# Block 0's up product one pair sooner, and penalties one pair in front of their use

## Chip, cores, metric

One core of a Trainium2 chip runs the program. The metric is the device time of one launch in microseconds (us); a median of 3 runs is given. Profiles are of one execution.

## What is computed

The reference has three stages. For B=2, H=8, S=576, D=64:

```python
scores = scale * np.matmul(q, k.transpose(0, 1, 3, 2))
kth = np.partition(scores, -top_k, axis=-1)[..., -top_k:-top_k + 1]   # top_k = 32
scores = np.where(scores >= kth, scores, -1000000000.0)
attn = softmax(scores); x = attn @ v            # to 1152 rows of 512
h = x @ w_in                                    # 512 x 2048
x = (h * np.cos(h)) @ w_out                     # 2048 x 512
expert_idx = np.argmax(x @ w_gate, axis=1)      # 8 experts, capacity 288 rows
h = np.maximum(disp @ w1[e], 0); y = h @ w2[e]  # per expert, 512 x 1024 x 512
out[i] = gate_w[i] * y[expert_idx[i], pos[i]]
```

(softmax is written out in the reference with a maximum, an exp and a division.)

## The kernel before

The rows are cut into 9 blocks of 128. A block of attention is 4 pairs of heads. Block 4 (`MIXED`) has rows of both batches. Each engine has a program of its own, one instruction stream written by hand; semaphores hold them together, and a wait holds everything behind it on its engine.

For a pair `p` of block `i` (a "tile" is one head, 128 x 576):

- PE makes the scores one block ahead (`scores`, L1205) in the bank `p_s`; ACT copies them to `s_sb` (L843).
- DVE finds the 32nd largest by four `max` and three `match_replace` per head (`pair_top`, L374, L377): 14 instructions a pair.
- POOL makes the biases (`bias`, L672); ACT the penalties (`pens`, L850); POOL subtracts them (`masks`, L678); ACT takes the exp (`exp_tile`, L862) into `probs`.
- PE transposes `probs` in three groups (`transpose_probs`, L1222, groups 0 to 11 in a block); ACT copies each to `probsT` (`copy_pT`, L870); PE multiplies with V (`times_v`, L1243) in `p_o`; after two pairs ACT copies `p_o` to `o_sb` (`copy_o`, L876).

Behind attention, and woven into it, each block goes through the up and the output product, one and two blocks late:

- DVE takes reciprocals of the row sums (`reciprocals`), POOL scales (`normalise`, L690), PE transposes x (`transpose_x`, L1253), ACT copies (`copy_xT`, L881).
- `up_half` (L1281) gives h in 4 chunks of 512 columns, two halves each; ACT reads every chunk twice (`copy_h`, L888, L889). POOL takes the fraction of a turn (`fraction`, L702 to L706), ACT the sine (`cosines`, L894), POOL the product (`gated`, L711), ACT casts its high part (`high_g`, L904), DVE subtracts for the low part (`low_g`, L404).
- `down_half` (L1303 to L1305) multiplies chunks of g with w_out in three passes of high and low parts. ACT and POOL split w_out in block 0 (`high_w_out` L910, `low_w_out` L717). Then y is copied, transposed and gated (`copy_y`, `copy_yT`, `copy_logits`).

In PE's block `i` the slots of the four pairs are filled thus by `part`: pair 0 has chunks 2 and 3 of the output product of block `i-2`, pairs 1 and 2 the four up chunks of block `i-1`, pair 3 output chunks 0 and 1 of block `i-1`. Block 0 has no such work, but two idle products a pair (`keep_warm`); block 1 has no part in pair 0. Exp and sine need different tables of ACT, so that a change between them is an `ACT_TABLE_LOAD`; copies, casts and the penalties' Relu take place under either. After the blocks come the routing and the experts, which the change does not touch.

Bodies called with `up=False` are block 0, with `down=False` block 1; the others are the loop's. In ACT the three are `first_body`, `second_body` and `body`.

Of the kernel before, what the change touches and what calls it, by code (L numbers as in the profile page):

```python
# [25 lines left out]
NBLK = NT // P  # L26
# [30 lines left out]
def build(nc, q_in_d, kt_in, v_in, w_in_d, w_out_d, wg_d, w1_d, w2_d, out):  # L57
    y_d = nc.dram_tensor("y_rows", (NBLK - 2, P, DM), F32, kind="Internal").ap()
    slots_d = nc.dram_tensor("slot_rows", (NSLOT, ROW), F32, kind="Internal").ap()
    with ExitStack() as ctx:  # L60
# [210 lines left out]
        def _(sp):  # L271
# [10 lines left out]

            next_queries(0)
            sp.dma_start(w_out, w_out_d).then_inc(w_out_loaded, 16)
# [73 lines left out]
        def _(dve):  # L358
# [48 lines left out]
            def body(i, up=True, down=True, mixed=False, batch=0, more=True):  # L407

                pair_top(i, 0)
                pair_top(i, 1)  # L410
                if up and not down:
                    reciprocals(i - 1)
                if down:
                    low_g(i - 2, 0)
                    low_g(i - 2, 1)
                pair_top(i, 2)
                if down:
                    low_g(i - 2, 2)
                    low_g(i - 2, 3)
                    reciprocals(i - 1)  # L420
                pair_top(i, 3)

            loops(dve, body)


# [231 lines left out]
        def _(pool):  # L657
# [62 lines left out]
            def body(i, up=True, down=True, mixed=False, batch=0, more=True):  # L720
                first, second = not up, up and not down
                if first:
                    for p in range(1, H // 2):
                        bias(i, p)
                        masks(i, p)
                        low_w_out(2 * p - 2)
                        low_w_out(2 * p - 1)
                    bias(i + 1, 0)
                    masks(i + 1, 0)
                    low_w_out(6)  # L730
                    low_w_out(7)
                    return
                if second:
                    normalise(i - 1)
                    bias(i, 1)
                    masks(i, 1)
                    bias(i, 2)
                    masks(i, 2)
                    fraction(i - 1, 0)
                    fraction(i - 1, 1)  # L740
                    bias(i, 3)
                    gated(i - 1, 0)
                    masks(i, 3)
                    gated(i - 1, 1)
                    fraction(i - 1, 2)
                    fraction(i - 1, 3)
                    gated(i - 1, 2)
                    bias(i + 1, 0)
                    gated(i - 1, 3)
                    masks(i + 1, 0)  # L750
                    bias(i + 1, 1)
                    masks(i + 1, 1)
                    bias(i + 1, 2)
                    return
                normalise(i - 1)
                masks(i, 2)
                bias(i, 3)
                fraction(i - 1, 0)
                masks(i, 3)
                fraction(i - 1, 1)  # L760
                if more:
                    bias(i + 1, 0)
# [4 lines left out]
                if more:  # L767
                    masks(i + 1, 0)
                    bias(i + 1, 1)
                gated(i - 1, 2)  # L770
                gated(i - 1, 3)
                if more:
                    masks(i + 1, 1)
                    bias(i + 1, 2)
# [63 lines left out]
        def _(act):  # L838
# [95 lines left out]
            def first_body(i):  # L934

                for p in range(1, H // 2):
                    copy_pT(i, 3 * p - 3)
                    copy_pT(i, 3 * p - 2)
                    scores(i + 1, p - 1)
                    if p == 3:  # L940
                        copy_o(i, 0)
                    copy_pT(i, 3 * p - 1)
                    pens(i, p)
                    exps(i, p)
                    high_w_out(2 * p - 2)
                    high_w_out(2 * p - 1)
# [6 lines left out]
                exps(i + 1, 0)  # L953
                high_w_out(6)
                high_w_out(7)

            def second_body(i):

                copy_pT(i, 0)
                copy_pT(i, 1)  # L960
                scores(i + 1, 0)
                copy_pT(i, 2)
                copy_xT(i - 1)
                pens(i, 1)
                exps(i, 1)

                copy_pT(i, 3)
                copy_pT(i, 4)
                scores(i + 1, 1)
                pens(i, 2)  # L970
                copy_pT(i, 5)
                copy_h(i - 1, 0)
                exp_tile(i, 4)
                copy_o(i, 0)
                copy_h(i - 1, 1)
                exp_tile(i, 5)

                copy_pT(i, 6)
                copy_pT(i, 7)
# [6 lines left out]
                high_g(i - 1, 0)  # L986
                high_g(i - 1, 1)
                exp_tile(i, 7)

                copy_h(i - 1, 3)  # L990
                copy_pT(i, 9)
                copy_pT(i, 10)
                cosines(i - 1, 1)
                scores(i + 1, 3)
                copy_pT(i, 11)
                pens(i + 1, 0)
                high_g(i - 1, 2)
                copy_o(i, 1)
                high_g(i - 1, 3)
                exps(i + 1, 0)  # L1000
                pens(i + 1, 1)

            def body(i, up=True, down=True, mixed=False, batch=0, more=True):

                first, second = not up, up and not down
                if first:
                    first_body(i)
                    return
                if second:
                    second_body(i)  # L1010
                    return
                copy_pT(i, 0)
                copy_pT(i, 1)
                exp_tile(i, 2)
                if more:
                    scores(i + 1, 0)
                copy_pT(i, 2)
                copy_xT(i - 1)
                exp_tile(i, 3)
                pens(i, 2)  # L1020
                if down:
                    copy_y(i - 2)
                copy_pT(i, 3)
                copy_pT(i, 4)
                exp_tile(i, 4)
# [6 lines left out]
                pens(i, 3)  # L1032
                if down:
                    copy_yT(i - 2)
                copy_o(i, 0)

                copy_h(i - 1, 1)
                copy_pT(i, 6)
                copy_pT(i, 7)
                exp_tile(i, 6)  # L1040
                cosines(i - 1, 0)
                copy_pT(i, 8)
                if more:
                    scores(i + 1, 2)
                copy_h(i - 1, 2)
                high_g(i - 1, 0)
                high_g(i - 1, 1)
                exp_tile(i, 7)

                copy_h(i - 1, 3)  # L1050
                copy_pT(i, 9)
                if more:
                    pens(i + 1, 0)
                cosines(i - 1, 1)
                copy_pT(i, 10)
                if more:
                    scores(i + 1, 3)
                copy_pT(i, 11)
                if more:
                    exp_tile(i + 1, 0)  # L1060
                high_g(i - 1, 2)
                if down:
                    copy_logits(i - 2)
                high_g(i - 1, 3)
                if more:
                    exp_tile(i + 1, 1)
                copy_o(i, 1)
                if more:
                    pens(i + 1, 1)
# [118 lines left out]
        def _(pe):  # L1188
# [145 lines left out]
            def body(i, keys, next_keys, up=True, down=True, mixed=False, batch=0, more=True):  # L1334
                def part(t, half):

                    if t < 2 and down:
                        down_half(i - 2, 2 + t, half)
                    if 2 <= t < 6 and up:
                        up_half(i - 1, t - 2, half)  # L1340
                    if t >= 6 and up:
                        down_half(i - 1, t - 6, half)

                for p in range(H // 2):
# [14 lines left out]
                    if p == 0 and up:  # L1359
# [199 lines left out]
```

## Time and profile before

| what | value |
|---|---|
| median of 3 runs | 661.59 us (660.81 to 661.72) |
| the profiled execution | 662.5 us, span 660.8 us |
| PE busy | 611.5 us, 93% |
| DVE busy | 526.6 us, 80% |
| ACT busy | 437.7 us, 66% |
| POOL busy | 289.7 us, 44% |

The table gives the sum of each engine's instructions over the span. It is a mean over the attention blocks (to about 440 us), the routing and the experts. The chain of waits is by 66% of the span on PE and by 15% on ACT.

### The profile page before, as it was taken

How to read it: one execution, taken by the hardware profiler on the slowest of the kernel's cores; microseconds unless marked ns; L12 is line 12 of the kernel's file. 1: busy time of each engine (PE TensorE's matmuls, PEld its weight loads, DVE VectorE, ACT ScalarE, POOL GpSimd, SP SyncE). 2: the span in 40 equal slices, each digit the busy share in tenths (PEclk: the TensorE clock that was granted, in tenths of full speed). 3: DMA queues.
4: the chain of work that ended last, by engine and by line, in shares of the span. 5: the costliest groups of instructions: out<-in, count | busy, mean ns of one | idle time of the engine just before them, and what ended most of it. 6: DMA issues, size and time to landing. Idle time of an engine off the chain costs nothing.

```text
span 660.8 us, 13481 instructions
## 1 busy us (share of the span) xinstructions
PE 611.5 (93%) x4302; PEld 548.3 (83%) x4302; DVE 526.6 (80%) x1017; ACT 437.7 (66%) x727; POOL 289.7 (44%) x294
## 2 busy tenths in 40 slices
PE   4778798899999999999999999999898999999994
PEld 3556696798897898998988978989687999999994
DVE  5999999988989979989989985016539877789751
ACT  2567478679679679688596796736438665667630
POOL 0376559457477366566474675821500111011111
PEclk9988599999999999999999999999899999999998
DMA  5874700000000000000000000060398675675400
GB/s 180 354 325 172 270 5 5 26 5 5 25 5 5 25 6 5 25 9 1 28 4 16 0 0 18 1 235 5 144 348 303 231 269 199 248 248 221 147 18 16
DMA packets 17792, 68.62 MB, mean 104 GB/s; under 512 B 1998, under 2 KB 6606, under 8 KB 15056
## 3 DMA queue, kind: packets, MB, share of 16 engines
q1 hardware_dynamic: 16000, 63.27, 25.8%
q0 software_dynamic: 1744, 4.73, 2.0%
q8 instruction: 27, 0.44, 0.3%
q14 instruction: 21, 0.17, 0.1%
HBM read 54.33 MB, written 14.45 MB: 104 GB/s over the span
## 4 chain that ended last, share of the span: by engine, by line
PE 66%; ACT 15%; POOL 8%; issue 7%; DVE 3%; DMA 0%; POOLq 0%; ACTq 0%; SPq 0%; DVEq 0%
PE p_a L1281 8%; PE p_o L1243 6%; PE p_b L1281 5%; PE p_s L1205 5%; PE p_b L1303 4%; PE p_t L1222 3%; PE p_s L1498 3%; PE p_b L1305 3%; PE p_b L1304 3%; PE p_t L1498 3%; PE p_t L1475 3%; POOL arena L678 3%; PE p_s L1475 3%; ACT arena L843 2%; POOL w_out_lo L717 2%
## 5 line engine op out<-in xcount | busy, mean ns | idle before, releaser
L374 DVE MAX8 top<-arena 128x8 f32<-128x576 f32 x288 | 201.1, 745 | 7.4 <-ACT arena L843 7.3
L377 DVE MATCH_REPLACE8 arena<-top,arena 128x576 f32<-128x576 f32 x216 | 158.6, 741 | 0.0
L678 POOL TENSOR_TENSOR arena<-arena,pen 128x576 f32<-128x576 f32 x72 | 100.7, 1421 | 57.1 <-ACT pen L850 57.1
L1243 PEld LDWEIGHTS p_o<-arena,probsT 128*128 128x128 f32 (+1 forms) x720 | 85.7, 191 | 12.8 <-ACT probsT L870 6.8
L1243 PE MATMUL p_o<-arena,probsT 128*128 128x65 f32 (+1 forms) x720 | 90.9, 273 | 5.6 <-ACT probsT L870 3.8
L870 ACT COPY probsT<-p_t 128x384 f32<-128x384 f32 x108 | 51.3, 480 | 53.9 <-PE p_t L1222 53.8
L1222 PE MATMUL p_t<-ident,arena 128*128 128x128 f32 x324 | 55.7, 284 | 13.2 <-ACT arena L862 13.2
L1281 PE MATMUL p_a<-xT,wff 128*128 128x128 f32 x512 | 66.0, 283 | 0.0
L1281 PE MATMUL p_b<-xT,wff 128*128 128x128 f32 x512 | 64.3, 279 | 0.0
L1303 PE MATMUL p_b<-w_out_lo,g_hi 128*128 128x512 f32 x144 | 62.5, 434 | 1.9 <-ACT h_sb L889 1.6
L1281 PEld LDWEIGHTS p_a<-xT,wff 128*128 128x128 f32 x512 | 60.8, 195 | 2.8 <-issue 2.4
L1222 PEld LDWEIGHTS p_t<-ident,arena 128*128 128x128 f32 x324 | 41.6, 148 | 24.7 <-ACT arena L862 17.8
L862 ACT ACTIVATE arena<-arena,biases 128x576 f32<-128x576 f32 x72 | 56.0, 779 | 9.1 <-POOL arena L678 8.3
L404 DVE TENSOR_TENSOR g_lo<-h_sb,g_hi 128x512 fp32r<-128x512 f32 x36 | 27.9, 811 | 42.0 <-ACT g_hi L904 41.6
L1281 PEld LDWEIGHTS p_b<-xT,wff 128*128 128x128 f32 x512 | 59.7, 192 | 0.3
L1205 PE MATMUL p_s<-arena,q_sb 64*128 64x160 f32 (+3 forms) x320 | 51.6, 476 | 8.4 <-DMA arena<-in_kt 4.3
L1305 PE MATMUL p_b<-w_out_hi,g_lo 128*128 128x512 f32 x144 | 56.7, 394 | 0.0
L1304 PE MATMUL p_b<-w_out_hi,g_hi 128*128 128x512 f32 x144 | 56.5, 392 | 0.0
L1205 PEld LDWEIGHTS p_s<-arena,q_sb 64*128 64x128 f32 (+1 forms) x320 | 36.8, 195 | 20.0 <-issue 17.0
L850 ACT ACTIVATE pen<-arena,biases 128x576 f32<-128x576 f32 x72 | 52.0, 776 | 1.6 <-POOL biases L672 1.6
L843 ACT COPY arena<-p_s 128x576 f32<-128x576 f32 x72 | 42.4, 644 | 14.2 <-PE p_s L1205 14.2
L711 POOL TENSOR_TENSOR h_sb<-h_sb,turns 128x512 f32<-128x512 f32 x32 | 40.5, 1285 | 23.0 <-ACT turns L894 23.0
(186 smaller groups left out, 1309.4 us busy)
## 6 DMA issues: line engine op xcount, KB each, us to landing
arena<-in_w SPq DMA_DIRECT2D x8, 2048.0 KB, 9.0
wff<-in_w SPq DMA_DIRECT2D x8, 2048.0 KB, 9.1
slot_rows<-y_now SPq DMA_DIRECT2D x1, 4626.0 KB, 14.7
wff<-in_w_out SPq DMA_DIRECT2D x1, 4096.0 KB, 12.2
wff<-in_w_in SPq DMA_DIRECT2D x1, 4096.0 KB, 22.0
wff<-slot_rows SPq DMA_DIRECT2D x8, 385.5 KB, 3.7
arena<-in_vones SPq DMA_DIRECT2D x2, 1300.0 KB, 16.8
q_sb<-in_q SPq DMA_DIRECT2D x36, 64.0 KB, 1.9
```

What stands on the lines that cost most here:

```text
L374: nc.vector.max(best, src).then_inc(top_step, 1)
L377: nc.vector.match_replace(work[:, a, :], best, src, LOWEST).then_inc(top_step, 1)
L678: nc.gpsimd.tensor_tensor(s_sb[:, t, :], s_sb[:, t, :], pen[:, t % 2, :], ALU.subtract).then_inc(masked, 1)
L843: nc.scalar.copy(s_sb[:, t, :], p_s[:, SPOT[t % 2]:SPOT[t % 2] + S]).then_inc(scores_copied, 1)
L862: nc.scalar.activation(probs[:, S * (t % 2):S * (t % 2) + S], s_sb[:, t, :], ACT.Exp, bias=biases[:, t, 0:1], scale=SCALE).then_inc(probs_ ...
L1205: last = mm(p_s[q, at + lo:at + hi], q_sb[d, p, q], kT[d, b, p, lo:hi], start=True, stop=True)
L1222: last = nc.tensor.transpose(p_t[:, at:at + P], probs[:, k:k + P], ident[:])
L1243: last = mm(p_o[q, lo:lo + n], probsT[:, g % 2, P * c + q.start:P * c + q.stop], vones[b][:, p, at:at + n], start=(k == 0), stop=(k == PAI ...
L1281: last = mm(bank_c[:, P * n:P * n + P], w_in[:, k, P * f:P * f + P], xT[:, k, :], start=(k == 0), stop=(k == KC - 1))
L1303: mm(p_b[:], g_hi[:, cols], w_out_lo[:, f, :], start=(f == 0), stop=False)
L1304: mm(p_b[:], g_hi[:, cols], w_out_hi[:, f, :], start=False, stop=False)
L1305: last = mm(p_b[:], g_lo[:, cols], w_out_hi[:, f, :], start=False, stop=(f == FC1 - 1))
```

## The change

Nothing is added or taken out: every engine has the same instructions in another order.

1. PE, block 1: the transpose of block 0's x stands first in the block, and up chunks 0 to 3 fill pairs 0 and 1; pair 2 has attention alone. Other blocks are as before.
2. ACT, POOL and DVE, all loop blocks: penalties, masks and top-k of a pair come one pair later against PE (`pens(i, 1)` to `pens(i, 3)` in pairs 0 to 2, `pens(i + 1, 0)` in pair 3), low parts and reciprocals one pair of top-k sooner. The sines stand before exp tile 6 and before the next block's exp tile 0.
3. Block 0: w_out is loaded before the queries of block 1, and its casts and low parts are shared out anew.

The core of the diff:

```diff
@@ sync
+            sp.dma_start(w_out, w_out_d).then_inc(w_out_loaded, 16)
             next_queries(0)
-            sp.dma_start(w_out, w_out_d).then_inc(w_out_loaded, 16)
@@ vector, loop body
                 pair_top(i, 0)
+                low_g(i - 2, 0)
+                low_g(i - 2, 1)
                 pair_top(i, 1)
...
+                low_g(i - 2, 2)
+                low_g(i - 2, 3)
+                reciprocals(i - 1)
                 pair_top(i, 2)
...
                 pair_top(i, 3)
@@ vector, block 1
+            pair_top(1, 0)
+            pair_top(1, 1, range(0, 2))
+            reciprocals(0)
+            pair_top(1, 1, range(2, 7))
@@ gpsimd, block 0
+                    low_w_out(0)
+                    low_w_out(1)
+                    bias(i, 1)
+                    masks(i, 1)
+                    low_w_out(2)
+                    low_w_out(3)
+                    bias(i, 2)
+                    masks(i, 2)
+                    bias(i, 3)
+                    masks(i, 3)
+                    low_w_out(4)
+                    low_w_out(5)
                     bias(i + 1, 0)
@@ gpsimd, block 1
                     normalise(i - 1)
+                    masks(i, 0)
+                    low_w_out(6)
+                    low_w_out(7)
@@ scalar, block 1
+                copy_xT(i - 1)
+                exps(i, 0)
...
                 copy_o(i, 0)
-                copy_h(i - 1, 1)
-                exp_tile(i, 5)
+                cosines(i - 1, 0)
+                exps(i, 2)
+                copy_h(i - 1, 2)
+                high_g(i - 1, 0)
+                high_g(i - 1, 1)
                 copy_pT(i, 6)
+                copy_h(i - 1, 3)
+                scores(i + 1, 2)
                 copy_pT(i, 7)
-                scores(i + 1, 2)
-                cosines(i - 1, 0)
                 pens(i, 3)
                 copy_pT(i, 8)
-                copy_h(i - 1, 2)
-                exp_tile(i, 6)
...
+                exps(i, 3)
@@ scalar, loop body
                 copy_pT(i, 7)
-                exp_tile(i, 6)
-                cosines(i - 1, 0)
-                copy_pT(i, 8)
                 if more:
                     scores(i + 1, 2)
+                pens(i, 3)
+                copy_pT(i, 8)
                 copy_h(i - 1, 2)
+                cosines(i - 1, 0)
+                exp_tile(i, 6)
                 high_g(i - 1, 0)
+                exp_tile(i, 7)
                 high_g(i - 1, 1)
...
@@ tensor
-                    if 2 <= t < 6 and up:
-                        up_half(i - 1, t - 2, half)
+                    c = t - 2 if down else t
+                    if 0 <= c < 4 and up:
+                        up_half(i - 1, c, half)
...
+                if up and not down:
+                    transpose_x(i - 1)
```

In the changed file the lines of the engines stand 7 to 11 further down.

ACT, pair 2 of block 4 (the same in all loop blocks), before: `p_t` copies are the transposes 6, 7 and 8, `arena<-arena,biases` is an exp tile, `turns<-turns` a sine.

```order
L870 COPY probsT<-p_t 128x384 x2
L862 ACTIVATE arena<-arena,biases 128x576
L894 ACT_TABLE_LOAD
L894 ACTIVATE turns<-turns 128x512 x2
L870 COPY probsT<-p_t 128x384
L843 COPY arena<-p_s 128x576 x2
L888 ACTIVATE turns<-p_a 128x512
L889 COPY h_sb<-p_a 128x512
L904 CAST g_hi<-h_sb 128x512 x2
L862 ACT_TABLE_LOAD
L862 ACTIVATE arena<-arena,biases 128x576
```

ACT, the same place in the changed kernel:

```order
L877 COPY probsT<-p_t 128x384 x2
L850 COPY arena<-p_s 128x576 x2
L857 ACTIVATE pen<-arena,biases 128x576 x2
L877 COPY probsT<-p_t 128x384
L895 ACTIVATE turns<-p_a 128x512
L896 COPY h_sb<-p_a 128x512
L901 ACT_TABLE_LOAD
L901 ACTIVATE turns<-turns 128x512 x2
L869 ACT_TABLE_LOAD
L869 ACTIVATE arena<-arena,biases 128x576
L911 CAST g_hi<-h_sb 128x512
L869 ACTIVATE arena<-arena,biases 128x576
```

The exp tile between transposes 7 and the sines (tile 6) stands behind the sines and a second table load now.

ACT, the end of block 4, before:

```order
L870 COPY probsT<-p_t 128x384
L850 ACTIVATE pen<-arena,biases 128x576 x2
L894 ACT_TABLE_LOAD
L894 ACTIVATE turns<-turns 128x512 x2
L870 COPY probsT<-p_t 128x384
L843 COPY arena<-p_s 128x576 x2
L870 COPY probsT<-p_t 128x384
L862 ACT_TABLE_LOAD
L862 ACTIVATE arena<-arena,biases 128x576
L904 CAST g_hi<-h_sb 128x512
```

ACT, the end of block 4 in the changed kernel:

```order
L877 COPY probsT<-p_t 128x384 x2
L850 COPY arena<-p_s 128x576 x2
L857 ACTIVATE pen<-arena,biases 128x576 x2
L937 COPY logits<-p_a 128x8
L877 COPY probsT<-p_t 128x384
L901 ACT_TABLE_LOAD
L901 ACTIVATE turns<-turns 128x512 x2
L869 ACT_TABLE_LOAD
L869 ACTIVATE arena<-arena,biases 128x576
L911 CAST g_hi<-h_sb 128x512
L883 COPY o_sb<-p_o 128x260
```

The copies of transposes 10 and 11 and the scores stood between the sines and the next block's exp tile 0; they are all in front of the sines now, and exp tile 0 comes straight behind them.

PE, start of block 1 before (`p_a<-ident,odd_whole` transposes x, `p_b<-arena` are the idle products of block 0):

```order
L1373 MATMUL p_b<-arena 128x512 x2
L1222 MATMUL p_t<-ident,arena 128x128 x3
L1205 MATMUL p_s<-arena,q_sb 128x160
L1205 MATMUL p_s<-arena,q_sb 128x416 x2
L1205 MATMUL p_s<-arena,q_sb 128x160
L1222 MATMUL p_t<-ident,arena 128x128 x3
L1243 MATMUL p_o<-arena,probsT 128x65 x3
L1222 MATMUL p_t<-ident,arena 128x128 x3
L1253 MATMUL p_a<-ident,odd_whole 128x128 x4
```

PE, start of block 1 in the changed kernel:

```order
L1384 MATMUL p_b<-arena 128x512 x2
L1260 MATMUL p_a<-ident,odd_whole 128x128 x4
L1229 MATMUL p_t<-ident,arena 128x128 x3
L1212 MATMUL p_s<-arena,q_sb 128x160
L1212 MATMUL p_s<-arena,q_sb 128x416 x2
L1212 MATMUL p_s<-arena,q_sb 128x160
L1288 MATMUL p_a<-xT,wff 128x128 x8
L1229 MATMUL p_t<-ident,arena 128x128 x3
L1250 MATMUL p_o<-arena,probsT 128x65 x3
L1288 MATMUL p_a<-xT,wff 128x128 x8
```

The transpose of x came behind three groups of transposes of `probs` and is the first thing of the block now, with the up product (`p_a<-xT,wff`) right behind the scores.

## Rows read from the trace of the kernel before

**Rows 1.** Busy time of one engine, page part 1: us, share, instructions.
```profile
PE 611.5 (93%) x4302; PEld 548.3 (83%) x4302; DVE 526.6 (80%) x1017; ACT 437.7 (66%) x727; POOL 289.7 (44%) x294
```

**Rows 2.** Busy time by stretch: length, then each engine, clock, DMA; blocks 5 and 8.
```profile
256.41:301.88 45.47, 45.07 (x334) 40.64 (x332) 41.44 (x86) 35.26 (x62) 28.28 (x29) 1.00 0.04 13
...
393.69:436.63 42.94, 41.07 (x305) 37.21 (x304) 14.43 (x31) 29.37 (x52) 26.45 (x32) 1.00 0.04 11
```

**Rows 3.** PE timeline, block 5, pairs 2 and 3: start us, us, instruction.
```profile
278.72 0.49 PE L1222 MATMUL p_t<-ident,arena 128*128 128x128 f32 x3
...
283.14 2.00 PE L1281 MATMUL p_a<-xT,wff 128*128 128x128 f32 x16
284.98 0.49 PE L1222 MATMUL p_t<-ident,arena 128*128 128x128 f32 x3
...
290.22 0.49 PE L1222 MATMUL p_t<-ident,arena 128*128 128x128 f32 x3
...
294.40 0.49 PE L1222 MATMUL p_t<-ident,arena 128*128 128x128 f32 x3
...
297.65 0.88 PE L1243 MATMUL p_o<-arena,probsT 128*128 128x65 f32 x6 [0.37 <-ACT probsT L870]
...
301.88 0.49 PE L1222 MATMUL p_t<-ident,arena 128*128 128x128 f32 x3
```

**Rows 4.** ACT timeline, the same stretch.
```profile
282.73 0.48 ACT L870 COPY probsT<-p_t 128x384 f32<-128x384 f32 x1 [2.35 <-PE p_t L1222]
...
283.90 1.28 ACT L894 ACT_TABLE_LOAD   x1
285.19 1.15 ACT L894 ACTIVATE turns<-turns 128x512 f32<-128x512 f32 x2
...
286.61 1.18 ACT L843 COPY arena<-p_s 128x576 f32<-128x576 f32 x2
287.67 0.62 ACT L888 ACTIVATE turns<-p_a 128x512 f32<-128x512 f32 x1
...
288.62 1.18 ACT L904 CAST g_hi<-h_sb 128x512 fp32r<-128x512 f32 x2
...
291.11 0.77 ACT L862 ACTIVATE arena<-arena,biases 128x576 f32<-128x576 f32 x1
...
293.11 1.46 ACT L850 ACTIVATE pen<-arena,biases 128x576 f32<-128x576 f32 x2
```

**Rows 5.** PE timeline before block 2.
```profile
79.69 3.25 PE L1281 MATMUL p_a<-xT,wff 128*128 128x128 f32 x16
...
103.64 0.55 PE L1222 MATMUL p_t<-ident,arena 128*128 128x128 f32 x3 [0.34 <-ACT arena L862]
...
117.50 0.55 PE L1222 MATMUL p_t<-ident,arena 128*128 128x128 f32 x3 [2.41 <-ACT arena L862]
```

**Rows 6.** DVE timeline, end of a pair of top-k and first low halves.
```profile
102.72 1.41 DVE L374 MAX8 top<-arena 128x8 f32<-128x576 f32 x2
104.24 1.71 DVE L404 TENSOR_TENSOR g_lo<-h_sb,g_hi 128x512 fp32r<-128x512 f32 x2
```

**Rows 7.** POOL timeline, end of block 0.
```profile
66.14 4.68 POOL L717 TENSOR_TENSOR w_out_lo<-wff,w_out_hi 128x1024 fp32r<-128x1024 f32 x2 [1.82 <-ACT w_out_hi L910]
70.78 1.05 POOL L690 TENSOR_TENSOR odd_whole<-o_sb,rden 128x512 f32<-128x512 f32 x1
```

**Rows 8.** ACT timeline, block 0.
```profile
23.06 0.46 ACT L870 COPY probsT<-p_t 128x384 f32<-128x384 f32 x1
...
59.95 0.38 ACT L876 COPY o_sb<-p_o 128x260 f32<-128x260 f32 x1 [0.97 <-PE p_o L1243]
```

**Rows 9.** Busy time by stretch of 4 us, columns as in rows 2.
```profile
40.00:44.00 4.00, 1.54 (x8) 0.62 (x6) 4.00 (x11) 2.55 (x4) 2.78 (x2) 1.00 1.00 419
44.00:48.00 4.00, 2.22 (x12) 1.44 (x11) 4.00 (x8) 3.64 (x7) 3.35 (x2) 0.59 0.49 183
```

**Rows 10.** DMA issues, page part 6: KB each, us to landing.
```profile
wff<-in_w_out SPq DMA_DIRECT2D x1, 4096.0 KB, 12.2
```

More of the change, by code:

```diff
@@ L405, in low_g, with body @@
                                         ALU.subtract).then_inc(g_lo_made, 1)
-            def body(i, up=True, down=True, mixed=False, batch=0, more=True):
+            def body(i):
                 pair_top(i, 0)
+                low_g(i - 2, 0)
+                low_g(i - 2, 1)
                 pair_top(i, 1)
[L411 to L415, printed above, removed]
+                low_g(i - 2, 2)
+                low_g(i - 2, 3)
+                reciprocals(i - 1)
                 pair_top(i, 2)
[L417 to L420, printed above, removed]
                 pair_top(i, 3)
-            loops(dve, body)
+            for p in range(H // 2):
+                pair_top(0, p)
+            pair_top(1, 0)
+            pair_top(1, 1, range(0, 2))
+            reciprocals(0)
+            pair_top(1, 1, range(2, 7))
+            pair_top(1, 2)
+            pair_top(1, 3)
+            with dve.Fori(2, NBLK) as i:
+                body(i)
             steps = [0]
@@ L767, in body @@
                 if more:
+                    bias(i + 1, 0)
                     masks(i + 1, 0)
-                    bias(i + 1, 1)
                 gated(i - 1, 2)
                 gated(i - 1, 3)
-                if more:
-                    masks(i + 1, 1)
-                    bias(i + 1, 2)
             pool.wait_ge(signs_ready, 2)
@@ L934, in first_body @@
             def first_body(i):
[L936 to L946, printed above, removed]
+                high_w_out(0)
+                high_w_out(1)
+                copy_pT(i, 0)
+                copy_pT(i, 1)
+                scores(i + 1, 0)
+                copy_pT(i, 2)
+                pens(i, 1)
+                exps(i, 1)
+                high_w_out(2)
+                high_w_out(3)
+                copy_pT(i, 3)
+                copy_pT(i, 4)
+                scores(i + 1, 1)
+                copy_pT(i, 5)
+                pens(i, 2)
+                exps(i, 2)
+                copy_o(i, 0)
+                copy_pT(i, 6)
+                copy_pT(i, 7)
+                scores(i + 1, 2)
+                copy_pT(i, 8)
+                pens(i, 3)
+                exps(i, 3)
+                high_w_out(4)
+                high_w_out(5)
                 copy_pT(i, 9)
@@ L952, in first_body @@
                 pens(i + 1, 0)
-                exps(i + 1, 0)
                 high_w_out(6)
@@ L1013, in body @@
                 copy_pT(i, 1)
-                exp_tile(i, 2)
                 if more:
                     scores(i + 1, 0)
+                pens(i, 1)
                 copy_pT(i, 2)
                 copy_xT(i - 1)
+                exp_tile(i, 2)
+                copy_y(i - 2)
                 exp_tile(i, 3)
-                pens(i, 2)
-                if down:
-                    copy_y(i - 2)
                 copy_pT(i, 3)
                 copy_pT(i, 4)
-                exp_tile(i, 4)
                 if more:
@@ L1061, in body @@
                 high_g(i - 1, 2)
-                if down:
-                    copy_logits(i - 2)
-                high_g(i - 1, 3)
+                copy_o(i, 1)
                 if more:
                     exp_tile(i + 1, 1)
-                copy_o(i, 1)
-                if more:
-                    pens(i + 1, 1)
+                high_g(i - 1, 3)
             for p in range(H // 2):
@@ L1358, in body @@
                     transpose_probs(i, g + 2)
-                    if p == 0 and up:
+                    if p == 0 and up and down:
                         transpose_x(i - 1)
```

76 lines of the change are left out of this document (32 added, 44 removed).

## The prediction

> **What bounds the kernel now.** I read the busy table of the page first, then the busy time by stretch, one stretch per block, then the timelines of PE and ACT in one block of the loop, and at last the timelines of the first 120 us. PE is busy 611.5 of 660.8 us [rows 1]. In a block of the loop it is busy 45.07 of 45.47 us at granted clock 1.00, while DVE, ACT and POOL have 41.44, 35.26 and 28.28 [rows 2]. So from block 2 to block 8 PE is the bound, and what counts is whether a wait is put in its way. The PE timeline of block 5 shows one: 0.37 us before a product with V at 297.65, released by ACT's copy of the probabilities [rows 3]. Pair 2 of that block lasts 11.50 us (278.72 to 290.22), pair 3 lasts 11.66 us (290.22 to 301.88), 11.3 without its wait. ACT is not the bound by its sum, but it runs in order, and each exp tile stands in front of a group of PE's transposes. In the old order exp tile 6, due at the start of pair 3, is computed before the table load for the sines, and exp tile 0 of the next block comes after sines that start five steps earlier in the pair. Before block 2 it is different: DVE is full, PE is often idle and half of the time at half clock [rows 9].
>
> **The steady blocks, step by step.** The work is the same in kind and count, four table loads per block among it. What moves is ACT's order. In pair 2 it is now: copy of transposes 8, reading of up chunk 2, table load, two sines, table load, exp tile 6. The transposes 8 end at 284.98 + 0.49, which is 6.75 us after the start of the pair [rows 3]. Just then ACT is free in the new order as well: ACT copies transposes 7 from 282.73 on, 4.0 us into the pair, and that copy (0.4), two score tiles (1.06) and two penalties (1.4) bring it to 6.8 [rows 4]. From there: copy 0.4, the two readings of an up chunk 1.05, load 1.28, sines 1.15, load 1.28, exp 0.78, all from [rows 4], sum 5.9. Exp tile 6 is ready at 12.7 us, PE asks for it at 11.5. **A wait of 1.25 us**, in each of blocks 2 to 7. In block 8 PE has no scores to make, so its pair is 1.2 us shorter and the wait about 2.2.
>
> At the end of pair 3 the order is now: copy of transposes 10, scores 3, the penalties of the next block, logits, copy of transposes 11, load, two sines, load, exp tile 0 of the next block. Transposes 10 end at 294.40 + 0.49, 4.7 us into the pair [rows 3]. Then 0.4 + 1.06 + 1.46 + 0.5 + 1.28 + 1.15 + 1.28 + 0.78 = 7.9 [rows 4]: ready at 12.6, asked for at 11.3. **A wait of 1.3 us** at the start of blocks 3 to 8, six times. The present wait of 0.37 us goes, since that copy stands before the sines now. Per block this is 1.25 + 1.3 - 0.37 = 2.2 us, and for blocks 2 to 7 it is +13.1 us. The blocks around the change of batch (3 and 4) have longer products with V, of which some 0.5 us fall into these waits: -0.5. Block 8: +2.2, and about +0.8 because the last sines now stand before the copy of the last output half, on which the last x depends, less 0.2 of the 1.9 us that PE idles there now [rows 2]: +2.8.
>
> The bounds of these terms. Below: if ACT's steps overlapped so that both chains came in time, 0 us per block and the 0.37 gone. Above: POOL's fraction steps and masks share the pairs, and if they came 0.5 us late at each of the two places, another +6 in sum. I take the sums of rows, since every link is a row of its own.
>
> DVE's order by itself is free: it has 41.44 of 45.47 us, now of 47.7, and the low halves, which now stand before top-k of pair 1 instead of pair 2, wait for the casts of g, not for DVE. POOL's sum is free too, but bias 3 comes behind two masks and two fractions now, and is ready about when ACT arrives for the penalties of pair 3. That is a tie without slack; hence the upper bound.
>
> **The first blocks.** The casts of w_out move up. SP issues its 4096 KB before its first wait; they land in 12.2 us [rows 10], and ACT wants them at 23.06 us [rows 8], with nine small loads in front. Price 0; if it were late, ACT would stand with the copies of block 0 behind it, 2 us at most. The queries of block 1 queue behind it, wanted 1 us later. Price 0, bound the same 2 us. Low halves 0 and 1 now stand before POOL's second bias; two of them take 4.7 us [rows 7], from 24.1 to 28.8, and hold that bias 0.3 us past the copy it is anyway behind: 0. DVE's reciprocals of block 0 move into the middle of pair 1; waiting for the copy of o_sb there costs DVE at most 0.5 us, which nobody asks for. Low halves 6 and 7 of w_out take POOL from 66.14 to 70.8 us now, and the x of block 0 waits for that [rows 7]. In the new order x comes first. Its input, the copy of o_sb at 59.95 [rows 8], comes some 1.5 us sooner, since no w_out step stands before the last bias. So x is ready near 60.4 instead of 71.8, two casts, the copy of xT and exp tile 0 follow on ACT, and PE starts block 1 at 63.7. The first up product is at about 66 instead of 79.69 [rows 5].
>
> But PE cannot keep these 14 us. Pairs 0 and 1 with two chunks each take 11.5 us each as in the loop, plus 1.5 to 3.5 us at half clock: the granted clock fell to 0.59 in the stretch after one with PE busy for 1.54 of 4 us [rows 9]. Pair 2 begins near 89 to 90. It has attention alone, 4.1 us of PE (11.5 less four up halves of 1.84, from 283.14 to 284.98 [rows 3]), but ACT has there load, two sines, load, two exps, two chunk readings, two casts, scores, penalties, copies and the exp of tile 6: 1.28 + 1.15 + 1.28 + 1.4 + 1.9 + 1.2 + 1.06 + 1.4 + 1.1 + 0.8 = 12.6 us [rows 4]. Pair 3 begins near 102, 1.6 us before the 103.64 of now [rows 5]. It takes 11.3 us, or up to 14.6 if the clock falls after the thin pair 2. Block 2 starts between 113.3 and 116.6 instead of 117.50. I take **-2 us**. The bounds: DVE reaches the low half of g a pair of top-k earlier (14 instructions at 0.7 us) than its 104.24 [rows 6], so the lead can't exceed some 9.5 us; and if the clock stays down longer, +1.
>
> **Sum.** 13.1 - 0.5 + 2.8 - 2 = +13.4 us. The profiled execution had 662.5 us; that makes 675.9. The median of the runs is 0.9 lower, so 675.0.
>
> A rule against the change stands in the Trainium skill (ScalarE: Activation LUTs, What ACT_TABLE_LOAD costs): a switch costs 1.28 us of load and about 1.38 of drain. By that rule, each of the two chains, with two loads, would be 2.8 us longer, and the kernel an estimated 33 us slower again, above 700. The rows show 1.28 us and then the first sine 1.29 after the load's start [rows 4], so I go by the rows; chance 0.01.
>
> **The rivals.**
> - *The lead is kept* (0.17). Block 2 starts 6 to 9.5 us early, limited by DVE. For it: DVE has no gap, and the new order asks for its results a pair later. Against: ACT's 12.6 us in a pair with 4.1 us of PE. Time: 675 - 4 to 7.5, that is 667.5 to 671.
> - *Faster* (0.08). Both exp tiles come in time, since PE's transposes 8 or the bias come sooner than I read, and the lead is kept as well. It decides at 4.7 us from transposes 8 to the end of exp tile 6, where I add up 5.9. Time: -9.5 - 6 x 0.37 = 650. With half a lead 655.
> - *More waits* (0.12). POOL is late with bias 3, or the casts of g come late for the output chunks, 0.5 to 1 us per block twice: 681 to 687.
> - *It cancels* (0.03): half of the waits and the full lead, near 661.
> - My forecast, both waits and a small lead: 0.59, 671 to 681.
>
> **Numbers.** The range goes from 666, which takes in the full lead with both waits, to 682. About 0.2% can be told from no change. Faster 0.08, same 0.03, slower 0.89.
>
> **What would show it.** In the profile after: block stretches of 47 to 48 us in place of 45.5 to 46.2; PE idle about 1.3 us before the transposes at the start of pair 3 and of pair 0, released by ACT's exp; no wait before the product with V behind transposes 10; the first up product near 66 us; block 2 starting at 113 to 117 us; the expert part as long as before. Wrong it would be if blocks keep 45.5 us, or block 2 starts before 110.

## The result, and the profile after

The changed kernel takes 689.01 us (median of 4 runs, 688.16 to 692.13) beside 661.65 us for the kernel before, measured beside it: a ratio of 1.0412, 95% interval 1.0385 to 1.0439. The profiled execution had 688.6 us, span 686.9 us. The sign was forecast, the size (675.0, at most 682) was not.

The page of the changed kernel, busy time and the chain of waits by engine; the first line answers to [rows 1]:

```profile
PE 620.8 (90%) x4302; PEld 555.0 (81%) x4302; DVE 526.7 (77%) x1017; ACT 440.4 (64%) x727; POOL 291.5 (42%) x294
...
PE 53%; ACT 14%; issue 13%; POOL 12%; DVE 5%; POOLq 1%; DVEq 1%; DMA 0%; ACTq 0%; SPq 0%
```

PE is busy 9.3 us longer with the same 4302 instructions, so some of them ran at a lower clock; the other 17 us of the longer span are time in which PE is idle. Its busy time by stretch, one stretch from the first transposes of a block to those of the next, for blocks 2, 3, 4, 5, 7 and 8 and for the rest (columns as in [rows 2]; the last stretch begins at the last transpose of x):

```profile
115.39:164.27 48.88, 45.20 (x333) 40.48 (x333) 40.15 (x83) 35.21 (x60) 28.51 (x29) 1.00 0.04 12
164.27:214.62 50.35, 46.62 (x364) 40.77 (x364) 41.73 (x86) 36.40 (x63) 28.69 (x31) 0.97 0.04 11
214.62:264.10 49.48, 47.87 (x404) 40.26 (x405) 42.75 (x86) 36.42 (x63) 28.46 (x30) 1.00 0.04 12
264.10:313.06 48.96, 45.20 (x333) 40.48 (x333) 42.07 (x87) 36.40 (x63) 29.15 (x30) 1.00 0.04 12
...
362.02:412.41 50.39, 46.72 (x332) 41.48 (x333) 41.73 (x86) 36.33 (x63) 28.56 (x30) 0.97 0.01 5
412.41:463.27 50.86, 44.25 (x301) 40.33 (x301) 23.97 (x50) 30.20 (x53) 26.75 (x34) 0.90 0.05 17
463.27:686.90 223.63, 209.06 (x1422) 198.36 (x1422) 151.27 (x248) 120.09 (x188) 29.27 (x25) 0.98 0.52 192
```

The same stretches of blocks 3, 4 and 8 in the kernel before, where [rows 2] has block 8 cut 0.6 us later:

```profile
163.02:208.84 45.82, 45.12 (x365) 39.93 (x364) 42.38 (x87) 36.01 (x63) 28.32 (x29) 1.00 0.04 13
208.84:256.41 47.57, 47.57 (x406) 40.23 (x405) 42.51 (x88) 36.92 (x64) 28.56 (x29) 1.00 0.04 13
...
393.69:436.03 42.34, 40.47 (x302) 36.79 (x300) 13.83 (x30) 29.37 (x52) 26.45 (x32) 1.00 0.03 9
```

Block 2 starts at 115.39 us, forecast 113.3 to 116.6 [rows 5]. From there a block takes 48.9 to 49.0 us, block 4 (rows of both batches) 49.5 us, blocks 3 and 7 50.4 us. Before, a block took 45.5 to 45.9 us and block 4 47.6 us. Of blocks 2 to 7 the granted clock is 0.97 in just blocks 3 and 7, and 1.00 in the others. Block 8 takes 50.9 us to the last transpose of x, 8.5 us more than before. What follows is no longer than before (223.6 us, before 224.8).

PE's timeline of block 5, pairs 2 and 3, the same place as [rows 3] (in brackets how long the engine was idle before an instruction, and which engine, tile and line released it):

```profile
286.46 0.49 PE L1229 MATMUL p_t<-ident,arena 128*128 128x128 f32 x3
...
292.73 0.49 PE L1229 MATMUL p_t<-ident,arena 128*128 128x128 f32 x3
...
299.58 0.55 PE L1229 MATMUL p_t<-ident,arena 128*128 128x128 f32 x3 [1.45 <-ACT arena L869]
...
303.74 0.49 PE L1229 MATMUL p_t<-ident,arena 128*128 128x128 f32 x3
...
308.51 0.80 PE L1250 MATMUL p_o<-arena,probsT 128*128 128x65 f32 x6
...
313.06 0.54 PE L1229 MATMUL p_t<-ident,arena 128*128 128x128 f32 x3 [2.30 <-ACT arena L869]
```

The pair-3 transposes come 13.12 us after those of pair 2 and waited 1.45 us for exp tile 6; the first transposes of the next block waited 2.30 us for exp tile 0. The wait before the product with V (297.65 in [rows 3]) is gone. These are the two waits that were forecast, at 1.25 and 1.3 us. ACT's timeline, the same stretch, which answers to [rows 4]:

```profile
292.20 1.44 ACT L857 ACTIVATE pen<-arena,biases 128x576 f32<-128x576 f32 x2 [0.17 <-POOL biases L677]
...
295.00 1.28 ACT L901 ACT_TABLE_LOAD   x1
296.29 1.15 ACT L901 ACTIVATE turns<-turns 128x512 f32<-128x512 f32 x2
297.46 1.28 ACT L869 ACT_TABLE_LOAD   x1
298.75 0.78 ACT L869 ACTIVATE arena<-arena,biases 128x576 f32<-128x576 f32 x1
...
304.26 0.48 ACT L877 COPY probsT<-p_t 128x384 f32<-128x384 f32 x1 [1.70 <-PE p_t L1229]
304.64 1.19 ACT L850 COPY arena<-p_s 128x576 f32<-128x576 f32 x2
306.50 1.44 ACT L857 ACTIVATE pen<-arena,biases 128x576 f32<-128x576 f32 x2 [0.68 <-POOL biases L677]
...
308.39 1.28 ACT L901 ACT_TABLE_LOAD   x1
309.69 1.15 ACT L901 ACTIVATE turns<-turns 128x512 f32<-128x512 f32 x2
310.86 1.28 ACT L869 ACT_TABLE_LOAD   x1
312.15 0.78 ACT L869 ACTIVATE arena<-arena,biases 128x576 f32<-128x576 f32 x1
```

Both chains are there link by link: load 1.28, sines 1.15, load 1.28, exp tile, in pair 2 behind the readings of h, in pair 3 behind the penalties and two short copies. But at 306.50 ACT had waited 0.68 us for POOL's bias. POOL's timeline of pair 3:

```profile
299.56 0.62 POOL L707 TENSOR_SCALAR odd_whole<-turns 128x512 f32<-128x512 f32 x1
...
305.01 1.30 POOL L711 TENSOR_TENSOR turns<-turns,odd_whole 128x512 f32<-128x512 f32 x1 [0.18 <-POOL odd_whole L709]
306.27 0.20 POOL L677 TENSOR_TENSOR biases<-top,signs 128x4 f32<-128x4 f32 x1
307.46 2.82 POOL L683 TENSOR_TENSOR arena<-arena,pen 128x576 f32<-128x576 f32 x2 [0.98 <-ACT pen L857]
```

The bias (306.27) comes behind two fractions (299.56 to 306.3), which themselves start behind the products of the pair before.

The waits of PE in block 8, and before the last transpose of x:

```profile
413.76 0.50 PE L1310 MATMUL p_b<-w_out_lo,g_hi 128*128 128x512 f32 x1 [0.80 <-DVE g_lo L404]
...
447.26 0.55 PE L1229 MATMUL p_t<-ident,arena 128*128 128x128 f32 x3 [2.22 <-ACT arena L869]
...
449.92 0.79 PE L1310 MATMUL p_b<-w_out_lo,g_hi 128*128 128x512 f32 x1 [1.32 <-ACT h_sb L896]
...
463.27 0.66 PE L1260 MATMUL p_a<-ident,odd_whole 128*128 128x128 f32 x4 [2.27 <-DVE odd_whole L512]
```

Four waits of 0.80, 2.22, 1.32 and 2.27 us, 6.6 us together where block 8 had 1.9 us before, and a granted clock of 0.90 over the block.

### The profile page after: what moved, and what is told of

The parts are those of the page before. It is cut to its first block, busy times and chain, and to the rows that moved or that the text cites. A ratio compares the mean times of both kernels' runs of the same rounds, so it can differ in the third digit from the quotient of the medians.

```text
span 686.9 us, 13728 instructions
## 1 busy us (share of the span) xinstructions
PE 620.8 (90%) x4302; PEld 555.0 (81%) x4302; DVE 526.7 (77%) x1017; ACT 440.4 (64%) x727; POOL 291.5 (42%) x294
## 4 chain that ended last, share of the span: by engine, by line
PE 53%; ACT 14%; issue 13%; POOL 12%; DVE 5%; POOLq 1%; DVEq 1%; DMA 0%; ACTq 0%; SPq 0%
PE p_a L1288 5%; PE p_s L1212 5%; PE p_o L1250 4%; PE p_b L1310 3%; PE p_s L1509 3%; PE p_t L1229 3%; PE p_t L1509 3%; PE p_b L1312 3%; PE p_b L1311 3%; PE p_t L1486 3%; POOL arena L683 3%; PE p_s L1486 3%; ACT pen L857 2%; ACT L901 2%; POOL turns L711 2%
## 5 line engine op out<-in xcount | busy, mean ns | idle before, releaser
L1229 PE MATMUL p_t<-ident,arena 128*128 128x128 f32 x324 | 58.2, 293 | 36.4 <-ACT arena L869 36.3
L1310 PE MATMUL p_b<-w_out_lo,g_hi 128*128 128x512 f32 x144 | 65.2, 453 | 2.1 <-ACT h_sb L896 1.3
L1212 PE MATMUL p_s<-arena,q_sb 64*128 64x160 f32 (+3 forms) x320 | 53.5, 492 | 8.4 <-DMA arena<-in_kt 4.3
L1312 PE MATMUL p_b<-w_out_hi,g_lo 128*128 128x512 f32 x144 | 58.8, 409 | 0.0
L1311 PE MATMUL p_b<-w_out_hi,g_hi 128*128 128x512 f32 x144 | 58.7, 408 | 0.0
L828 POOL DMA_INDIRECT out_rows<-turns,own_number x8 | 9.2, 1150 | 94.2 <-DVE turns L601 93.0
```

The costliest lines, as they stand in the source:

```text
L1212: last = mm(p_s[q, at + lo:at + hi], q_sb[d, p, q], kT[d, b, p, lo:hi], start=True, stop=True)
L1229: last = nc.tensor.transpose(p_t[:, at:at + P], probs[:, k:k + P], ident[:])
L1310: mm(p_b[:], g_hi[:, cols], w_out_lo[:, f, :], start=(f == 0), stop=False)
L1311: mm(p_b[:], g_hi[:, cols], w_out_hi[:, f, :], start=False, stop=False)
L1312: last = mm(p_b[:], g_lo[:, cols], w_out_hi[:, f, :], start=False, stop=(f == FC1 - 1))
```

## The experiments

**The start by itself** (`new_start`). Blocks 0 and 1 of the change, the old loop behind them. Beside what the diff of the change has for these blocks, the second bodies end as the old ones did, and DVE makes block 2 in an order between the two:

```diff
@@ vector
+            pair_top(2, 0)
+            low_g(0, 0)
+            low_g(0, 1)
+            pair_top(2, 1)
+            pair_top(2, 2)
+            low_g(0, 2)
+            low_g(0, 3)
+            reciprocals(1)
+            pair_top(2, 3)
@@ gpsimd, end of block 1
+                    bias(i + 1, 1)
+                    masks(i + 1, 1)
+                    bias(i + 1, 2)
@@ scalar, end of block 1
+                pens(i + 1, 1)
```

> Blocks 0 and 1 of the change (all engines, the w_out load first), the old loop from block 2 on, with DVE's low halves of block 0 in their new places. My theory: the blocks of the loop cost the 27 us, and the start by itself gives what the trace of the change shows at the first transposes of block 2, 115.4 instead of 117.5 us: 659.5, 2 us faster than before. Rival, the start also carries a loss that shows later (penalties and top-k of block 2 come late in the old loop): 662 to 665.

Measured: 662.04 us, ratio 0.9999 (0.9982 to 1.0016). Block 2 began even earlier than forecast and PE waited for the low half at once:

```profile
109.80 0.55 PE L1256 MATMUL p_t<-ident,arena 128*128 128x128 f32 x3 [1.18 <-ACT arena L887]
...
115.64 0.77 PE L1337 MATMUL p_b<-w_out_lo,g_hi 128*128 128x512 f32 x1 [4.12 <-DVE g_lo L404]
```

The lead of 7.7 us was there, and 4.1 us of it went in one wait. Behind that wait PE was busy all the time, but at half clock:

```profile
115.64:120.00 4.36, 4.36 (x15) 3.67 (x15) 4.33 (x11) 0.79 (x2) 1.58 (x2) 0.50 0.00 0
```

At 157.61 us, before a product with V in pair 3, PE was 1.2 us ahead of the same place before (158.79). So the start neither costs nor gives anything by itself; the gain that I expected (2 us) is not there, and neither is the rival's loss (the kernel before took 662.33 us beside it).

**The loop by itself** (`new_loop`): the old blocks 0 and 1 in front of the new loop, and nothing at their end for pair 1 and 2 of block 2.

```diff
@@ gpsimd, end of block 1
-                    bias(i + 1, 1)
-                    masks(i + 1, 1)
-                    bias(i + 1, 2)
@@ scalar, end of block 1
-                pens(i + 1, 1)
```

> The old blocks 0 and 1 with the new order of the loop from block 2 on. My theory: all of the loss is here, so 2 us more than the change: 690 to 692. Rival, a part of the loss comes from how block 1 hands over to block 2: 680 or less.

Measured: 693.95 us in one run, 2 us above what I expected. The same waits stand in its trace at the same places (1.48 and 2.31 us in block 5). All of the loss is in the loop's order. From block 2 to the last transpose of x this profile is 3.0 us longer than the one of the change. Its waits there are no longer, but the clock was 0.97 in four of blocks 2 to 7 instead of two.

**An exp tile in front of the sines** (`exp6_first`, `exp0_first`).

```diff
@@ exp6_first, scalar, pair 2
+                exp_tile(i, 6)
                 cosines(i - 1, 0)
-                exp_tile(i, 6)
@@ exp0_first, scalar, pair 3
+                if more:
+                    exp_tile(i + 1, 0)
                 cosines(i - 1, 1)
-                if more:
-                    exp_tile(i + 1, 0)
```

> The change with exp tile 6 in front of the first two sines, nothing else. By the prediction's step (PE waits at pair 3 for that tile alone) the 1.45 us before the transposes of pair 3 go, 7 times: 679. Rival: the sines and the reading of the last up chunk come late as well, and the wait moves to the output product that stands behind them in pair 3: same time within 3 us, and PE waits there 1.5 to 2 us a block, released by the copy of h or the low half of g.

> The change with exp tile 0 of the next block in front of the last two sines, nothing else. By the prediction's step the 2.3 us at the start of a block go, 6 times: 675. Rival: the wait moves to output chunk 2 in pair 0, behind the low half of g: same time within 3 us.

Measured: 695.61 and 694.77 us, one run each, 6.6 and 5.8 us above the median of the change. In each, PE no longer waits for the tile that was moved; it waits at the next output product instead, in block 5 of `exp6_first` here, with what is left of the wait at the start of the next block:

```profile
305.58 0.80 PE L1310 MATMUL p_b<-w_out_lo,g_hi 128*128 128x512 f32 x1 [2.70 <-ACT h_sb L896]
...
317.64 0.54 PE L1229 MATMUL p_t<-ident,arena 128*128 128x128 f32 x3 [1.09 <-ACT arena L869]
```

and at the start of block 6 of `exp0_first` here:

```profile
315.73 0.50 PE L1310 MATMUL p_b<-w_out_lo,g_hi 128*128 128x512 f32 x1 [2.75 <-DVE g_lo L404]
```

2.7 us each, longer than the wait that went (1.45 and 2.30 us). The sum of a block's waits grew less: 3.8 us in `exp6_first` and 4.5 in `exp0_first`, beside 3.75 in the change. The rivals had the mechanism right: what is late is the whole chain with the sines, and whichever tile is put in front of it, the other work behind it (the reading of the last up chunk, the low half of g) becomes what PE waits for. The time was outside their "within 3 us". In `exp6_first` most of the excess is clock: it was 0.93 to 0.97 in every block from 2 to 8, and PE was busy 5.4 us longer there than in the change. In `exp0_first` it is 3.7 us of waits in these blocks, and a later part (routing and experts) that took 3.6 us longer, which the edit doesn't touch.

**The table loads taken away** (`no_sine`, and `before_no_sine` as the control). The sine is replaced by a copy, so that the blocks need one table.

```diff
-                nc.scalar.activation(part, part, ACT.Sin, scale=TURN)
+                nc.scalar.activation(part, part, ACT.Copy, scale=TURN)
```

> The change with ACT's Copy in place of the sine, so that the blocks have no table load. It leaves out the cosine: g is h times the angle, and so the routing of rows to experts can differ; only the blocks (to the last transpose of x) are to be read. My theory: ACT's chain between two exp tiles is 2.6 us shorter at both places, both waits go, and a loop block takes 45 to 45.5 us in place of 48.9 to 50.4. Rival: the new order holds PE also without the loads (POOL's biases and fractions): 47 us or more.

> The kernel before with the same replacement, cosine left out, as the control for no_sine: its blocks keep 45 to 46 us, since PE waits for ACT less than half a microsecond a block there.

Measured: 658.16 and 651.46 us. Read from the transpose of x in block 2 to that in block 8, six blocks: 113.97 to 392.73 is 46.5 us a block with the new order, 120.06 to 390.11 is 45.0 with the old. With the sines the same places give 49.7 (121.25 to 419.57) and 46.1. So of 3.6 us that the new order costs per block, 2.2 hang on the table loads (and on what they do to the clock, which was 1.00 in both kernels without sines) and 1.4 to 1.5 do not. I had expected 45 to 45.5; the rival had a part. What is left is mostly one wait a block, in pair 0 before output chunk 2 (one run each):

```profile
295.91 0.50 PE L1310 MATMUL p_b<-w_out_lo,g_hi 128*128 128x512 f32 x1 [1.08 <-DVE g_lo L404]
```

and POOL's timeline ahead of it shows where the lateness comes from:

```profile
288.84 0.20 POOL L677 TENSOR_TENSOR biases<-top,signs 128x4 f32<-128x4 f32 x1
290.03 2.81 POOL L683 TENSOR_TENSOR arena<-arena,pen 128x576 f32<-128x576 f32 x2 [0.99 <-ACT pen L857]
292.80 2.51 POOL L716 TENSOR_TENSOR h_sb<-h_sb,turns 128x512 f32<-128x512 f32 x2
```

The masks of the next block's pair 0 stand in front of the product for g chunk 2 (292.80), as they did in the old order. New is that their bias comes as late as 288.84, behind two fractions: the penalties wait for it and the masks for the penalties (0.99), and so all behind them is late.

**The bias alone** (`bias_early`).

```diff
@@ gpsimd
                 gated(i - 1, 1)
+                if more:
+                    bias(i + 1, 0)
                 fraction(i - 1, 2)
                 fraction(i - 1, 3)
                 if more:
-                    bias(i + 1, 0)
                     masks(i + 1, 0)
```

> The change with POOL's bias of the next block in front of fractions 2 and 3. In the changed kernel ACT waits 0.68 us for it before the penalties in pair 3, and that is in the chain to exp tile 0. My theory: 0.6 us less at the start of blocks 3 to 8, 685. Rival: the bias then waits for DVE and holds the fractions, no gain or slower, 688 to 691.

Measured: 684.19 us in one run, 4.8 us below the change. The wait at the start of a block went from 2.30 to 1.55 us:

```profile
309.73 0.55 PE L1230 MATMUL p_t<-ident,arena 128*128 128x128 f32 x3 [1.55 <-ACT arena L870]
```

This is close to the 1.3 us of the prediction, so the term that was missing there is POOL's bias. Over the six block starts the waits went from 12.2 to 8.5 us. The clock stayed up as well; block 7, which had 0.97 in the change:

```profile
357.93:406.05 48.12, 45.17 (x333) 40.55 (x333) 41.73 (x86) 36.24 (x63) 28.45 (x30) 1.00 0.01 5
```

In all, blocks 2 to 7 take 6.9 us less than in the change, 3.7 of it waits and 3.2 PE's busy time; a start 0.5 us later and a last part 2.0 us longer take some of it back. That the clock followed from the shorter waits is argued from one profile of each.

**The clock** (`fill`): two idle products in the place of the wait at the start of a block.

```diff
@@ tensor, end of a block
+                if down and more:
+                    wait(pe, logits_copied, i - 1)
+                    for _ in range(2):
+                        mm(p_a[:], kT[:, 0, 0, 0:P], kT[:, 0, 0, 0:512], start=True, stop=True)
```

> The change with two idle products (1.9 us at full clock) at the end of each block from 2 on, in the place where PE waits 2.2 us for exp tile 0; they write a bank that nobody reads then. My theory: after that wait the granted clock falls in some blocks (0.97 over blocks 3 and 7, half speed in their first 2 us), and with the wait filled it stays at 1.00 there: 3 us less in the loop, 684 to 687. Rival: the clock falls for the other waits as well, or the products end too late and hold the transposes: 689 or more.

Measured: 682.28 us (679.6 to 688.28), ratio 1.0346 (1.0303 to 1.0390), where the change has 1.0412 (1.0385 to 1.0439). Blocks 3, 7 and 8 of it:

```profile
158.83:207.61 48.78, 46.77 (x369) 40.56 (x369) 41.73 (x86) 36.42 (x63) 28.67 (x31) 1.00 0.04 12
...
355.61:404.50 48.89, 46.92 (x336) 41.22 (x337) 41.73 (x86) 36.32 (x63) 28.60 (x30) 1.00 0.01 5
404.50:453.27 48.77, 42.96 (x301) 39.38 (x301) 23.98 (x50) 30.21 (x53) 26.77 (x34) 0.93 0.07 19
```

Blocks 3 and 7 take 48.8 and 48.9 us at clock 1.00 instead of 50.4 at 0.97: more work on PE, and less time. The other blocks from 2 to 7 have 1.00 too. Block 8 has no such products in front of its later waits and stays at 0.93. The medians alone would not settle it: the two intervals touch, and one of the four runs took 688.28 us. The profile is of the fastest run (679.6), in which block 2 also began at 109.9 us, which is no effect of the products (below). Of the 9.0 us between the two profiles, 2.5 are in blocks 2 to 7 (I had expected 3) and 2.1 in block 8.

**Can the lead be kept?** (`new_start2`, `new_start3`). Two other handovers to the old loop.

```diff
@@ new_start2, vector, block 2, against new_start
             pair_top(2, 1)
-            pair_top(2, 2)
             low_g(0, 2)
             low_g(0, 3)
             reciprocals(1)
+            pair_top(2, 2)
@@ new_start3, gpsimd, against new_start2: end of block 1, and block 2
-                    bias(i + 1, 2)
...
                 normalise(i - 1)
+                if isinstance(i, int) and i == 2:
+                    bias(i, 2)
                 masks(i, 2)
```

> As new_start, but in block 2 DVE makes low halves 2 and 3 of block 0 and the reciprocals of block 1 before top-k of pair 2. In new_start block 2 began at 109.8 us, 7.7 us before the old kernel, and lost it at the first output product of that block, where PE waited 4.1 us for low half 2. My theory: that wait goes and 4 to 6 us of the lead stay: 656 to 658. Rival: the penalties of pair 2 come late then, because top-k of pair 2 does, and PE waits in pair 1 or 2 instead: 660 to 662.

> As new_start2, with POOL's bias of pair 2 of block 2 behind the x of block 1. In new_start2 that bias stood in front of x and waited for DVE's top-k of pair 2, and PE waited 5.3 us for x. My theory: with both handovers right the lead at block 2 (110 to 115 us instead of 117.5) stays up to the end: 655 to 659, faster than before. Rival: top-k of pair 2 ends near 118 us, the penalties and exps of pair 2 hold ACT in pairs 0 and 1, and nothing is left: 661 to 663.

Measured: 666.94 us, ratio 1.0072 (1.0046 to 1.0098), and 661.58 us, ratio 0.9994 (0.9962 to 1.0025). The first is slower than both my theory and its rival had it, the second is the rival's. In `new_start2` the wait for low half 2 went and one for x came, since POOL's bias of pair 2 stood in front of x and waited for DVE:

```profile
126.25 1.11 PE L1287 MATMUL p_a<-ident,odd_whole 128*128 128x128 f32 x4 [5.29 <-POOL odd_whole L708]
```

In `new_start3` (where POOL makes block 2 in front of its loop) both are right, and PE waits later, at output chunk 0 of block 1 and then at chunk 2:

```profile
153.63 0.77 PE L1346 MATMUL p_b<-w_out_lo,g_hi 128*128 128x512 f32 x1 [3.43 <-DVE g_lo L404]
...
166.65 0.50 PE L1346 MATMUL p_b<-w_out_lo,g_hi 128*128 128x512 f32 x1 [1.81 <-DVE g_lo L404]
```

In the kernel before, DVE is busy at least 19.85 of every 20 us from 20 to 140 us, so what counts is whether DVE loses time. In `new_start3` it does, in front of the first low halves:

```profile
110.78 2.68 DVE L404 TENSOR_TENSOR g_lo<-h_sb,g_hi 128x512 fp32r<-128x512 f32 x2 [4.17 <-ACT g_hi L938]
```

It stood still for 4.2 us (6.2 in `new_start2`) until ACT had cast g, and was full again from 120 to 160 us. So the reading that fits is that DVE's lead is spent there, and the old loop, which asks for its top-k a pair sooner, then waits for DVE. No run tests this by itself. Neither kernel is faster than the one before.

**The order of the loads** (`w_out_first`), alone on the kernel before.

```diff
@@ sync
+            sp.dma_start(w_out, w_out_d).then_inc(w_out_loaded, 16)
             next_queries(0)
-            sp.dma_start(w_out, w_out_d).then_inc(w_out_loaded, 16)
```

> The kernel before with the load of w_out in front of the queries of block 1, nothing else. My theory: both are in time either way, so no difference that can be told, within 0.2%. Rival: the queries queue behind 4 MB and PE's scores of block 1 come late: 1 to 2 us slower.

Measured: 662.12 us, ratio 1.0013 (0.9993 to 1.0033). No difference that can be told, as the price of 0 had it.

## Why the prediction was right and where it was wrong

The two waits and their mechanism were forecast. The size was not: the sum of +13.4 us stands against +26.1 us of span in the two profiles, that is -2.1 at the start, +20.8 in blocks 2 to 7, +8.5 in block 8 and -1.1 behind it. Three steps failed: the chain to exp tile 0, block 8, and the price of a wait.

- **Start, -2: right in the profile by some luck, and worth nothing.** 115.39 us instead of 117.50. Pair 2 of block 1 began at 92.88 (forecast 89 to 90) and pair 3 at 101.31 (near 102). But the time was not spent as described: PE waited 3.2 us for the exp tiles behind the sines in front of pair 2, which then took 8.4 us and not 12.6. The clock fell (0.55 over 100 to 105 us), and pair 3 took 14.1 us (up to 14.6). Eight profiles with this start code begin block 2 at 109.8 to 115.9 us (below), so that one of them proves little. And the term stood for a lasting gain, of which `new_start` shows none.
- **Wait for exp tile 6, 1.25 us a block: right.** 1.44 to 1.51 us in blocks 2, 3, 5, 6 and 7, 0.70 in block 4, 2.22 in block 8 (forecast 2.2). For blocks 2 to 7 that is 8.0 us, 7.5 in the sum. By the prediction's own rows it would have been 12.7 - 11.5 = 1.2.
- **Wait for exp tile 0, 1.3 us a block: too small.** 2.2 to 2.3 us, 0.91 at the end of block 4, together 12.2 us where the sum had 7.8. The step that failed is "Then 0.4 + 1.06 + 1.46 + ...": it let ACT go from the scores to the penalties at once. I had looked for a late bias in pair 2 and called it a tie, and there it was one (0.17 us at 292.20). The bias of pair 3, behind two fractions, was not looked at, and came 0.68 us late. `bias_early` gives it back.
- **Block 8, +2.8: measured +8.5.** The wait for tile 6 is as forecast. Three more waits had no or too small a term: 0.80 us for the low half of g at its start, 1.32 for the reading of the last up chunk and 2.27 for the last x, the last two against 0.66 and 0.19 before. In all the idle time grew by 4.7 us (6.6 beside 1.9). The other 3.8 us are PE's busy time, 44.25 beside 40.47, at a granted clock of 0.90.
- **The clock, put at nothing.** I priced each wait at its own length. But PE's busy time rose by 1.5 us in block 3 (46.62 beside 45.12) and in block 7, by 3.4 us in blocks 2 to 7 together and by 3.8 in block 8: about 7 us. I had allowed for a lower clock in the thin pair of block 1 alone. `fill` tells this apart from the waits.

Blocks 2 to 7 add up: waits of 8.0 + 12.2, less the 2.8 us that PE was idle there before, and 3.4 of busy time, give 20.8, as measured (115.39 to 412.41 beside 117.50 to 393.69). The range missed since its upper end held late POOL work of 6 us and neither the clock nor block 8. The nearest rival was "more waits", 681 to 687, and it too was short.

Two readings of the trace before were off, and neither bears on the sum: a block took up to 47.6 us (block 4) and not up to 46.2, and before block 2 the mean granted clock is 0.88, so PE was not half of the time at half clock; [rows 9] shows two stretches only.

The load of tables cost what the rows showed: from the load's start to the first sine 1.29 us (295.00 to 296.29). The Trainium skill (ScalarE: Activation LUTs, What ACT_TABLE_LOAD costs) adds a drain to each switch. The trace does not show it: what stands behind a load starts 1.29 or 1.30 us after the load's start wherever it does not wait for another engine.

What stays open is whether a loop exists that asks for top-k a pair later, as this one does, and still starts its sines in time, as the old one does. It may be what a lasting lead of the start needs; it wasn't tried. Open is also why the clock fell behind some waits and not behind others of the same length.

## What to carry to other kernels

When an in-order engine serves a saturated one, price a moved step by the chain from the last thing it needs to the first thing that is waited for, and do this for every consumer behind it: moving one of them in front of the late step moved the wait here, and the waits of a block did not get shorter in sum. Follow the chain into every other queue that feeds it, the small instruction behind two long ones above all. And where PE is the bound, a wait can cost more than its length, as the clock may fall behind it (about 7 of 26 us here), so that filling it with idle products can be cheaper than leaving it.

## What was not expected of the hardware

The granted clock behind a wait of 2.2 to 2.3 us differed between blocks that were otherwise the same. In front of blocks 6 and 7 PE waited 2.30 us each time; over block 6 the clock stayed at 1.00, over block 7 it was 0.97, with 0.66 over its first 5 us (362 to 367 us), that is the 1.2 GHz level for a part of them: it was 0.83 over the first 2 us and 0.50 over the next two. Other profiles of the new loop order show the same scatter: of blocks 2 to 7, the clock was below 1.00 in four in `new_loop`, in two in `exp0_first`, and in all six in `exp6_first`. It was below it in none of them in `bias_early`, whose longest wait there was 1.56 us, nor in `fill`, with 1.49 us.

And the start code of the change, the same but for the handover at its end, began block 2 anywhere from 109.8 to 115.9 us in eight profiles with the sines. The difference goes with the clock in pairs 2 and 3 of block 1. First the change over 90 to 110 us, then `new_start`:

```profile
90.00:110.00 20.00, 15.53 (x72) 12.21 (x72) 18.01 (x36) 15.88 (x27) 13.07 (x14) 0.74 0.03 8
```

```profile
90.00:110.00 20.00, 16.74 (x96) 13.40 (x97) 20.00 (x42) 18.41 (x32) 13.60 (x15) 0.92 0.03 7
```

0.74 in the one and 0.92 in the other, for the same code up to there. The two profiles with 0.92 (`new_start` and `fill`) began block 2 at 109.8 and 109.9 us, the six with 0.74 at 113.7 to 115.9 us. So a lead of 5 us at one place of one profile can be luck of the clock; the medians of several runs tell, and they told of no gain.
